# Second mixture of experts: three moves of work in VectorE's, ScalarE's and SyncE's orders

## The chip, the cores and the metric

The kernel runs on one core of a Trainium2 chip. The metric is the device time of one launch in microseconds (us), the median of several runs. The engines are TensorE (PE; its weight loads are shown as PEld), VectorE (DVE), ScalarE (ACT), GpSimd (POOL) and SyncE (SP), which here only issues DMAs. A name with a q behind it (DVEq, PEldq, SPq) is the instruction sequencer of that engine. "L1170" is line 1170 of the kernel.

## The reference

Three stages follow each other. An attention over q, k, v (2 x 8 heads x 768 positions x 64) gives x of 1536 rows x 512. A first mixture adds four experts over all rows, `p[:, e] * (relu(x @ w1[e]) @ w2[e])`, hidden size 1024. The second mixture is sparse:

```
skip_score = x @ w_skip;  do_compute = skip_score > 0;  out = x.copy()
logits = xc @ w_gate;     e_idx = argmax(logits);  gate_w = softmax(logits)[e_idx]
for e in range(8):
    h = relu(xc[mask] @ w1[e]);  y[mask] = gate_w[mask] * (h @ w2[e])
out[do_compute] = xc + y
```

So about half of the rows go to one of 8 experts each, and which row goes where is known only at run time. Everything is float32.

## The kernel before, in words

The change touches the second mixture alone. During the last group of the first mixture the kernel chooses an expert per row and scatters one entry per chosen row (its number and gate weight) into a list in DRAM (`send_entries`, L575, POOL, 12 indirect DMAs). The list has columns of 64 entries, and each is one tile; a tile is of one expert. This input gives 14 tiles: experts 0 to 3 have one tile each, expert 4 five (tiles 4 to 8), experts 5 and 6 one each, expert 7 three (tiles 11 to 13). Each tile holds its 64 rows as 128 half rows.

A tile's work goes through the engines as follows:

- POOL gathers the rows of tile i by an indirect DMA from `x1_rows` (L579) into one of six buffers `xg`, and later scatters the finished rows to `out` (L583). Behind the scatter of tile i stands the gather of tile i+5.
- DVE copies gathered rows into `x_in` (`rows_in`, L1175), PE transposes them (`next_rows`, L1488), and DVE copies the transposed rows to `xt2` (`copy_x`, L1136).
- PE multiplies by the expert's first weights (`layer1`, L1506), ACT applies the relu (`relu_h`, L788), PE transposes the result (`turn_h`, L1513), ACT copies it (`copy_ht`, L792), PE multiplies by the second weights (`layer2`, L1529).
- DVE adds the result, times the gate, to the rows (`add_x`, L1170).

PE works a tile ahead. Its turn i is: `layer1` of tile i, `next_rows` of tile i+1, `layer2` of tile i-1, `turn_h` of tile i. `layer1` of tile i waits for `copy_x(i)` and for its expert's first weights in slot 0.

Weights of an expert are 8 pieces of 512 KB, 4 for each layer. SP loads them (L437) into slot 0 (expert 0) or one of three further slots, and counts each layer that has arrived in `set_ready` (`arrived`, L441). Before use they are copied into slot 0 (`place`): DVE copies 2 of 4 pieces of layer 1 and 3 of 4 of layer 2 (L1188), ACT the others (L799). DVE's turn i before the change is: `add_x(i)`; `place` of layer 2 if tile i+1 has another expert than tile i; the row numbers of tile i+6 (`make_ids`, L1163 to L1165, read from the list); two register loads from a table (L1178, L1181); and, if there are further tiles, `copy_x(i+2)`, `place` of layer 1 if tile i+2 has another expert than tile i+1, and `rows_in(i+3)`. All engines take their instructions in the order written, and a wait holds up all behind it.

At the start of this stage SP issues: all of set 0, layer 1 of set 1, one piece of its layer 2; then (once the last rows of the first mixture are there, `keep(G-1)`, L422) the write of these rows to `x1_rows`, from which POOL gathers tile 0; the three other pieces of set 1; after `gathered[0]` the write of the same rows to `out` (`send_out(G-1)`, L427), two pieces of set 2; after `gathered[1]` everything else. The list, once all entries have landed, is loaded from DRAM by ACT (L784), ahead of ACT's relu of tile 0. `make_ids(1)` on DVE and by it the gather of tile 1 wait for the list.

Of the kernel before, what the change touches and what calls it, by code (L numbers as in the profile page):

```python
# [18 lines left out]
def sparse_attention_moe_moe(nc, q, k, v, dprobs, w1, w2, w_skip, w_gate, v1, v2, out):  # L19
# [27 lines left out]
    NT = N // P  # L47
    G = 4
# [4 lines left out]
    SIDES = 2  # L53
    QT = P // SIDES
    LISTS = N // QT
    TILES = (N + E2 * (QT - 1)) // QT
    SLOTS = 6
# [7 lines left out]
    PIECES = 4  # L65
# [28 lines left out]
    route_list = nc.dram_tensor("route_list", (QT * COLS, 2), F32).ap()  # L94
# [5 lines left out]
    with ExitStack() as ctx:  # L100
# [3 lines left out]
        def sem(name):  # L104
            return ctx.enter_context(nc.semaphore(name))
# [104 lines left out]
        lst = a1[:, o:o + 2 * COLS].rearrange("p (c e) -> p c e", e=2)  # L210
# [34 lines left out]
        def keys_of(a):  # L245
# [23 lines left out]
        x1_out, x1_kept = sem("x1_out"), sem("x1_kept")  # L269
        x1_last = sem("x1_last")  # L270
        x1_tr, x1t_ok, logit_ok = sem("x1_tr"), sem("x1t_ok"), sem("logit_ok")
        r_dve, shifted, r_exp, hot_ok, sum_ok, rank_ps, count_ps = (
            sem("r_dve"), sem("shifted"), sem("r_exp"), sem("hot_ok"), sem("sum_ok"), sem("rank_ps"), sem("count_ps"))
        entry_ok, entries_out, list_in, table_ok = (
            sem("entry_ok"), sem("entries_out"), sem("list_in"), sem("table_ok"))
# [7 lines left out]
        r1_done, relu_ok, ht_done, ht_ok, r2_done, y_ok = (  # L283
            sem("r1_done"), sem("relu_ok"), sem("ht_done"), sem("ht_ok"), sem("r2_done"), sem("y_ok"))
# [10 lines left out]
        def _(sp):  # L295
# [42 lines left out]
            def w1_piece(src, c):  # L338
                return src[c * P:(c + 1) * P, :]

            def w2_piece(src, c):
                return src[2 * c * P:2 * (c + 1) * P, :].rearrange("(j p) d -> p j d", p=P)

            def two(dst):
                return dst.rearrange("p (j d) -> p j d", j=2)
# [72 lines left out]
            def keep(g):  # L418

                sp.wait_ge(acc_ok, 2 + GR * (G * (E1 - 1) + g + 1))  # L420
                rows, src = rows_of_group(g)
                sp.dma_start(x1_rows[rows].rearrange("(t p) d -> p t d", p=P), src).then_inc(x1_kept, 16)  # L422

            def send_out(g):

                rows, src = rows_of_group(g)
                sp.dma_start(out[rows].rearrange("(t p) d -> p t d", p=P), src).then_inc(x1_out if g < G - 1 else x1_last, 16)  # L427

            def slot_of(e):
                return 1 + (e - 1) % AHEAD if e else 0  # L430

            def load_set(e, layer, pieces=range(PIECES)):

                for c in pieces:
                    dst = wset[:, slot_of(e), (PIECES * layer + c) * PIECE:(PIECES * layer + c + 1) * PIECE]
                    src = w2_piece(v2[e], c) if layer else w1_piece(v1[e], c)
                    sp.dma_start(two(dst) if layer else dst, src).then_inc(set_in[slot_of(e)][layer], 16)  # L437

            def arrived(e, layer):
                sp.wait_ge(set_in[slot_of(e)][layer], 16 * PIECES * (1 + (e - 1) // AHEAD))  # L440
                sp.sem_inc(set_ready, 1)  # L441
# [18 lines left out]
            load_set(0, 1)  # L460
            load_set(1, 0)

            load_set(1, 1, range(1))
            keep(G - 1)
            load_set(1, 1, range(1, PIECES))
            arrived(1, 0)
            sp.wait_ge(gathered[0], 16)
            send_out(G - 1)
            load_set(2, 0, range(2))
            arrived(1, 1)  # L470

            sp.wait_ge(gathered[1], 16)
            load_set(2, 0, range(2, PIECES))
# [9 lines left out]
            tiles = sp.value_load(table[0:1, 0:1], min_val=1, max_val=TILES)  # L483
# [139 lines left out]
        def _(act):  # L623
# [133 lines left out]
            def route_exp(g):  # L757
                act.wait_ge(shifted, g + 1)
                nc.scalar.activation(t8[1][:, g * GR:(g + 1) * GR, :], t8[0][:, g * GR:(g + 1) * GR, :], ACT.Exp).then_inc(r_exp, 1)


            for g in range(G):
                c = G * (E1 - 1) + g
# [11 lines left out]
            for t in range(GR * (G - 1), NT):  # L775
                route_copy(t)
            route_exp(G - 1)

            act.wait_ge(x1_kept, 16 * (G - 1))
            act.wait_ge(x1_out, 16 * (G - 1))  # L780
            act.wait_ge(x1_tr, NT)
            act.wait_ge(entries_out, 16 * NT)
            for j in range(SIDES):
                act.dma_start(lst[j * QT:(j + 1) * QT, :, :].rearrange("p c e -> p (c e)"), route_list.rearrange("(p c) e -> p (c e)", p=QT)).then_inc(list_in, 16)  # L784

            def relu_h(i):
                act.wait_ge(r1_done, i + 1)
                nc.scalar.activation(h2, ps[:, 0, 0:FQ], ACT.Relu).then_inc(relu_ok, 1)  # L788
# [23 lines left out]
            tiles = act.value_load(table[0:1, 0:1], min_val=1, max_val=TILES)  # L812
# [20 lines left out]
        def _(dve):  # L833
# [265 lines left out]
            e = E1 - 1  # L1099
# [5 lines left out]
            for g in range(G):  # L1105
                c = G * e + g
# [27 lines left out]
            def copy_x(i):  # L1134
                dve.wait_ge(x_tr, i + 1)
                nc.vector.tensor_copy(xt2, ps[:, 4, 0:DQ]).then_inc(x_ok, 1)  # L1136
# [25 lines left out]
            def make_ids(i, k):  # L1162
                col = dve.value_load(table[0:1, bass.ds(i + COL_OF, 1)], min_val=0, max_val=COLS - 1)  # L1163
                nc.vector.tensor_scalar(id_of[:, k:k + 1], lst[:, bass.ds(col, 1), 0], side[:, 0:1], None, ALU.add).then_inc(id_ok, 1)
                nc.vector.tensor_copy(gate_of[:, k:k + 1], lst[:, bass.ds(col, 1), 1]).then_inc(gate_ok, 1)  # L1165

            def add_x(i, k):
                dve.wait_ge(r2_done, i + 1)
                dve.wait_ge(gate_ok, i)
                nc.vector.scalar_tensor_tensor(out=xg[k % SLOTS], in0=ps[:, 2, 0:DQ], scalar=gate_of[:, k:k + 1], in1=xg[k % SLOTS],  # L1170
                                               op0=ALU.mult, op1=ALU.add).then_inc(y_ok, 1)

            def rows_in(k, uses):
                dve.wait_ge(gathered[k % SLOTS], 16 * uses)
                nc.vector.tensor_copy(x_in, xg[k % SLOTS]).then_inc(rows_ok, 1)  # L1175

            def set_at(i):
                return dve.value_load(table[0:1, bass.ds(i + SET_OF, 1)], min_val=0, max_val=E2 - 1)  # L1178

            def waits_at(i):  # L1180
                return dve.value_load(table[0:1, bass.ds(i + WAIT_OF, 1)], min_val=0, max_val=AHEAD)  # L1181

            def place(then, at, layer):

                dve.wait_ge(set_ready, 2 * then + 1 + layer)
                for c in range(W2_DVE if layer else W1_DVE):
                    cols = slice((PIECES * layer + c) * PIECE, (PIECES * layer + c + 1) * PIECE)
                    nc.vector.tensor_copy(wset[:, 0, cols], wset[:, bass.ds(at, 1), cols].rearrange("p o c -> p (o c)")).then_inc(  # L1188
                        w2_by_dve if layer else w1_by_dve, 1)

            dve.wait_ge(table_ok, 1)
            tiles = dve.value_load(table[0:1, 0:1], min_val=1, max_val=TILES)
# [22 lines left out]
            fourth, at_fourth = set_at(3), waits_at(3)  # L1215
            def turn(i, ago, now, then, at_now, at_then):

                add_x(i, i)
                with dve.If(ago < now):
                    place(now, at_now, 1)  # L1220
                make_ids(i + SLOTS, i + SLOTS)
                beyond, at_beyond = set_at(i + 3), waits_at(i + 3)
                if i + 1 < TILES:
                    with dve.If(tiles > i + 1):

                        copy_x(i + 2)
                        with dve.If(now < then):
                            dve.wait_ge(r1_done, i + 2)
                            place(then, at_then, 0)
                        rows_in(i + 3, 1 + (i + 3) // SLOTS)  # L1230
                        turn(i + 1, now, then, beyond, at_then, at_beyond)
            turn(1, second, third, fourth, at_third, at_fourth)


# [360 lines left out]
```

## Time and profile before

| | before |
|---|---|
| median of 3 runs | 815.03 us (813.95 to 815.23) |
| profiled execution | 812.8 us, span 811.1 us |
| PE busy | 743.6 us, 92% of the span |
| DVE busy | 286.5 us, 35% |
| ACT busy | 204.6 us, 25% |
| POOL busy | 68.5 us, 8% |
| mean granted TensorE clock | 0.972 |

The second mixture takes the span from about 630 us on. "Busy" is the time in which an instruction of the engine was running; the granted clock is 1.00 at TensorE's full 2.4 GHz and 0.50 at 1.2 GHz, and a value between is a mean over a stretch.

### The profile page before, as it was taken

To read this page: it belongs to the slowest core of one execution; us is meant where nothing else is said; L and a number is where in the kernel's file an instruction comes from. 1 tells how busy PE (TensorE), PEld (TensorE's weight loads), DVE (VectorE), ACT (ScalarE), POOL (GpSimd) and SP (SyncE) were. 2 spreads that over 40 slices of the span, in tenths; PEclk is the share of its full clock that TensorE was granted. 3 is DMA by queue.
4 is the path that set the end of the run, shared out by engine and by line. 5 is a ranking of instruction groups with operands and counts; after the bars stand their busy time and mean duration, and the time that the engine had idled before them with its cause. 6 is when DMAs were issued, how large, how long until landed. Compare 5 with 4: busy or idle time off the path is not lost.

```text
span 811.1 us, 12549 instructions
## 1 busy us (share of the span) xinstructions
PE 743.6 (92%) x4608; PEld 608.9 (75%) x4609; DVE 286.5 (35%) x818; ACT 204.6 (25%) x498; POOL 68.5 (8%) x97
## 2 busy tenths in 40 slices
PE   5699999999999999999999999999998778778675
PEld 4588888989989899898898998989897333333233
DVE  4987664524222122341121432232322542211421
ACT  3654454523211011230110311202020132112210
POOL 2530000000000000000000000010101331211210
PEclk9899999999999999999999999999999698999898
DMA  9893612103220000330000020202029599920000
GB/s 206 197 218 88 131 43 57 44 34 108 99 72 1 1 0 0 104 104 0 0 0 0 31 72 1 78 1 78 33 80 344 179 363 396 399 100 19 8 2 19
DMA packets 76947, 75.22 MB, mean 93 GB/s; under 512 B 54088, under 2 KB 54364, under 8 KB 76512
## 3 DMA queue, kind: packets, MB, share of 16 engines
q1 hardware_dynamic: 74080, 69.72, 27.9%
q0 software_dynamic: 2656, 4.66, 1.9%
q8 instruction: 27, 0.44, 0.2%
q10 hardware_dynamic: 160, 0.20, 0.1%
q14 instruction: 24, 0.20, 0.1%
HBM read 66.82 MB, written 8.24 MB: 93 GB/s over the span
## 4 chain that ended last, share of the span: by engine, by line
PE 87%; DVE 5%; issue 2%; DVEq 2%; ACT 1%; DMA 1%; POOL 0%; ACTq 0%; SPq 0%; POOLq 0%
PE ps L1241 22%; PE ps L1243 22%; PE ps L1242 22%; PE ps L1506 7%; PE ps L1529 7%; PE ps L1303 1%; PE ps L1275 1%; PE ps L1426 1%; PE ps L1289 1%; DVE sets L1188 1%; PE ps L1254 1%; PE ps L1416 1%; DVE acc L887 1%; DVEq L1181 1%; DVEq L1163 1%
## 5 line engine op out<-in xcount | busy, mean ns | idle before, releaser
L1241 PE MATMUL ps<-xt_hi,w_hi 128*128 128x384 f32 (+1 forms) x508 | 173.0, 341 | 0.0
L1243 PE MATMUL ps<-xt_hi,w_lo 128*128 128x384 f32 (+1 forms) x508 | 170.2, 335 | 0.0
L1242 PE MATMUL ps<-xt_lo,w_hi 128*128 128x384 f32 (+1 forms) x508 | 170.1, 335 | 0.0
L707 ACT ACTIVATE h_hi<-ps 128x384 fp32r<-128x384 f32 x128 | 63.0, 492 | 359.1 <-PE ps L1243 358.9
L1241 PE MATMUL ps<-w_hi,h_hi 128*128 128x512 f32 x384 | 151.7, 395 | 0.0
L1243 PE MATMUL ps<-w_hi,h_lo 128*128 128x512 f32 x384 | 150.0, 391 | 0.0
L1242 PE MATMUL ps<-w_lo,h_hi 128*128 128x512 f32 x384 | 149.8, 390 | 0.0
L933 DVE SCALAR_TENSOR_TENSOR h_lo<-ps,h_hi 128x384 fp32r<-128x384 f32 x128 | 71.1, 556 | 167.1 <-ACT h_hi L707 166.9
L1241 PEld LDWEIGHTS ps<-xt_hi,w_hi 128*128 128x128 f32 x508 | 95.4, 188 | 1.7 <-issue 0.8
L1242 PEld LDWEIGHTS ps<-xt_lo,w_hi 128*128 128x128 f32 x508 | 95.5, 188 | 0.5
L1243 PEld LDWEIGHTS ps<-xt_hi,w_lo 128*128 128x128 f32 x508 | 95.4, 188 | 0.0
L1506 PE MATMUL ps<-sets,acc 128*64 128x512 f32 x224 | 61.3, 699 | 34.4 <-DVE sets L1188 17.8
L1243 PEld LDWEIGHTS ps<-w_hi,h_lo 128*128 128x128 f32 x384 | 72.1, 188 | 15.2
L1241 PEld LDWEIGHTS ps<-w_hi,h_hi 128*128 128x128 f32 x384 | 72.1, 188 | 15.0 <-issue 0.8
L1242 PEld LDWEIGHTS ps<-w_lo,h_hi 128*128 128x128 f32 x384 | 72.2, 188 | 14.1
L944 DVE SCALAR_TENSOR_TENSOR acc<-ps,dp,acc 128x512 f32<-128x512 f32 x36 | 27.0, 750 | 140.4 <-PE ps L1243 140.3
L1506 PEld LDWEIGHTS ps<-sets,acc 128*64 128x64 f32 x224 | 17.5, 157 | 69.4 <-issue 48.0
L1529 PE MATMUL ps<-sets,acc 128*64 128x256 f32 x448 | 53.3, 392 | 1.5 <-issue 0.7
L575 POOL DMA_INDIRECT route_list<-entry,slot x12 | 12.1, 1004 | 451.5 <-DVE entry L1096 449.1
L1529 PEld LDWEIGHTS ps<-sets,acc 128*64 128x64 f32 x448 | 32.6, 141 | 18.5 <-issue 4.6
L1170 DVE SCALAR_TENSOR_TENSOR acc<-ps,gate_of,acc 128x256 f32<-128x256 f32 x13 | 6.3, 483 | 97.4 <-PE ps L1529 97.4
L788 ACT ACTIVATE h_rows<-ps 128x512 f32<-128x512 f32 x14 | 8.4, 597 | 90.3 <-PE ps L1506 75.6
(172 smaller groups left out, 623.3 us busy)
## 6 DMA issues: line engine op xcount, KB each, us to landing
sets<-in_moe_w SPq DMA_DIRECT2D x64, 512.0 KB, 7.7
stage<-in_moe_w SPq DMA_DIRECT2D x24, 512.0 KB, 4.0
stage<-in_k SPq DMA_DIRECT2D x16, 192.0 KB, 4.8
acc<-in_v SPq DMA_DIRECT2D x4, 768.0 KB, 6.5
x_rows<-acc SPq DMA_DIRECT2D x4, 768.0 KB, 4.2
out_rows<-acc SPq DMA_DIRECT2D x4, 768.0 KB, 5.1
acc<-in_moe_w POOLq DMA_DIRECT2D x4, 512.0 KB, 4.3
acc<-in_moe_w SPq DMA_DIRECT2D x4, 512.0 KB, 5.7
```

The costliest lines, as they stand in the source:

```text
L575: nc.gpsimd.indirect_dma_start(route_list, bass.IndirectOffsetOnAxis(slot[:, t:t + 1], 0), entry[:, t, :], None, bounds_check=QT * COLS - ...
L707: nc.scalar.activation(h_hi[:, f, :], ps[:, f % 2, 0:GT], ACT.Relu).then_inc(h_hi_ok, 1)
L788: nc.scalar.activation(h2, ps[:, 0, 0:FQ], ACT.Relu).then_inc(relu_ok, 1)
L887: TT(rows[0:VR, 0:left], rows[0:VR, 0:left], rows[0:VR, left:2 * left], ALU.add).then_inc(vsum_step, 1)
L933: nc.vector.scalar_tensor_tensor(out=h_lo[:, f, :], in0=ps[:, f % 2, 0:GT], scalar=0.0, in1=h_hi[:, f, :].bitcast(F32), op0=ALU.max, op1=A ...
L944: nc.vector.scalar_tensor_tensor(out=acc[:, t, :], in0=bank, scalar=dp[:, t, bass.ds(e, 1)], in1=acc[:, t, :], op0=ALU.mult, op1=ALU.add). ...
L1163: col = dve.value_load(table[0:1, bass.ds(i + COL_OF, 1)], min_val=0, max_val=COLS - 1)
L1241: mm(dst, a_hi, b_hi, start=start, stop=False)
L1242: mm(dst, a_hi, b_lo, start=False, stop=False)
L1243: return mm(dst, a_lo, b_hi, start=False, stop=stop)
L1506: last = mm(ps[j * QT:(j + 1) * QT, 0, 0:FQ], xt2[:, from_c:from_c + QT], wset[:, 0, at:at + FQ], start=(c == 0), stop=(c == KC - 1))
L1529: last = mm(ps[j * QT:(j + 1) * QT, 2, 0:DQ], ht2[:, at:at + QT], wset[:, 0, to:to + DQ], start=(f == 0), stop=(f == FC - 1))
```

## The change

Three edits. On SP, two pieces of set 1's layer 2 instead of one are issued ahead of `keep(G-1)`; two pieces of set 2 are issued behind `arrived(1, 0)`, ahead of the wait for the first gather; and SP loads the list, behind `send_out(G-1)`. ACT loads it no more. On DVE, the block with `copy_x(i+2)`, `place` of layer 1 and `rows_in(i+3)` stands ahead of `add_x(i)`, in an If of its own.

```
--- before
+++ after
             load_set(1, 0)
 
-            load_set(1, 1, range(1))
+            load_set(1, 1, range(2))
             keep(G - 1)
-            load_set(1, 1, range(1, PIECES))
+            load_set(1, 1, range(2, PIECES))
             arrived(1, 0)
+            load_set(2, 0, range(2))
+            arrived(1, 1)
             sp.wait_ge(gathered[0], 16)
             send_out(G - 1)
-            load_set(2, 0, range(2))
-            arrived(1, 1)
+
+            sp.wait_ge(x1_kept, 16 * (G - 1))
+            sp.wait_ge(x1_out, 16 * (G - 1))
+            sp.wait_ge(x1_tr, NT)
+            sp.wait_ge(entries_out, 16 * NT)
+            for j in range(SIDES):
+                sp.dma_start(lst[j * QT:(j + 1) * QT, :, :]..., route_list...).then_inc(list_in, 16)
 
             sp.wait_ge(gathered[1], 16)
             load_set(2, 0, range(2, PIECES))
...
             route_exp(G - 1)
-
-            act.wait_ge(x1_kept, 16 * (G - 1))
-            act.wait_ge(x1_out, 16 * (G - 1))
-            act.wait_ge(x1_tr, NT)
-            act.wait_ge(entries_out, 16 * NT)
-            for j in range(SIDES):
-                act.dma_start(lst[j * QT:(j + 1) * QT, :, :]..., route_list...).then_inc(list_in, 16)
-
             def relu_h(i):
...
             def turn(i, ago, now, then, at_now, at_then):
 
+                with dve.If(tiles > i + 1):
+                    copy_x(i + 2)
+                    with dve.If(now < then):
+                        dve.wait_ge(r1_done, i + 2)
+                        place(then, at_then, 0)
+                    rows_in(i + 3, 1 + (i + 3) // SLOTS)
+
                 add_x(i, i)
                 with dve.If(ago < now):
                     place(now, at_now, 1)
...
                 if i + 1 < TILES:
                     with dve.If(tiles > i + 1):
-
-                        copy_x(i + 2)
-                        with dve.If(now < then):
-                            dve.wait_ge(r1_done, i + 2)
-                            place(then, at_then, 0)
-                        rows_in(i + 3, 1 + (i + 3) // SLOTS)
                         turn(i + 1, now, then, beyond, at_then, at_beyond)
```

## Rows read from the trace of the kernel before

**Rows 1.** The page: the chain that ended last, by engine.
```profile
PE 87%; DVE 5%; issue 2%; DVEq 2%; ACT 1%; DMA 1%; POOL 0%; ACTq 0%; SPq 0%; POOLq 0%
```

**Rows 2.** Timeline of PE: start us, us, line, operation, count [idle before, released by].
```profile
657.59 3.65 PE L1506 MATMUL ps<-sets,acc 128*64 128x512 f32 x16 [0.82 <-DVE sets L1188]
669.22 5.35 PE L1506 MATMUL ps<-sets,acc 128*64 128x512 f32 x16 [3.42 <-DVE sets L1188]
695.27 3.65 PE L1506 MATMUL ps<-sets,acc 128*64 128x512 f32 x16 [2.84 <-DVE acc L1136]
702.83 0.66 PE L1513 MATMUL ps<-ident,h_rows 128*128 128x128 f32 x4
706.32 5.35 PE L1506 MATMUL ps<-sets,acc 128*64 128x512 f32 x16 [2.84 <-DVE acc L1136]
718.72 3.65 PE L1506 MATMUL ps<-sets,acc 128*64 128x512 f32 x16 [2.50 <-DVE acc L1136]
740.64 5.35 PE L1506 MATMUL ps<-sets,acc 128*64 128x512 f32 x16 [3.00 <-DVE sets L1188]
754.31 5.35 PE L1506 MATMUL ps<-sets,acc 128*64 128x512 f32 x16 [3.76 <-DVE sets L1188]
791.06 3.65 PE L1506 MATMUL ps<-sets,acc 128*64 128x512 f32 x16 [2.47 <-DVE acc L1136]
```

**Rows 3.** Chain of waits, 701 to 707 us: start us, us, what.
```profile
702.94 0.08 DVE acc L1170
703.02 0.49 issue
...
703.51 0.30 DVEq L1163
...
705.76 0.43 DVE acc L1136
```

**Rows 4.** Chain of waits, pieces of one turn of PE.
```profile
695.27 3.65 PE ps L1506 x16
698.92 0.37 PE ps L1488 x2
699.29 3.63 PE ps L1529 x32
```

**Rows 5.** Stretches: us, busy PE PEld DVE ACT POOL (count), clock, DMA share, GB/s.
```profile
706.30:711.70 5.40, 5.38 (x17) 1.61 (x18) 0.09 (x1) 0.00 (x0) 0.36 (x1) 0.68 1.04 394
718.70:722.40 3.70, 3.68 (x17) 1.19 (x18) 0.09 (x1) 0.00 (x0) 0.72 (x1) 1.00 0.12 37
660.00:715.00 55.00, 42.52 (x252) 19.22 (x250) 13.10 (x33) 11.99 (x16) 9.98 (x9) 0.91 1.02 389
```

**Rows 6.** Timeline of all engines, 660 to 684 us (the weights of tiles 3 and 4).
```profile
666.91 2.00 ACT L799 ACTIVATE sets<-sets 128x1024 f32 x2 [5.03 <-SPq L441]
...
677.96 2.00 ACT L799 ACTIVATE sets<-sets 128x1024 f32 x2 [2.75 <-SPq L441]
678.47 0.66 PE L1513 MATMUL ps<-ident,h_rows 128*128 128x128 f32 x4
678.99 1.88 DVE L1188 COPY sets<-sets 128x1024 f32 x3
681.78 1.30 DVE L1188 COPY sets<-sets 128x1024 f32 x2
683.00 0.27 DVE L1175 COPY acc<-acc 128x256 f32<-128x256 f32 x1
```

**Rows 7.** PE's sequencer, line 1534, 701 to 707 us: register loads, first and last start.
```profile
L1534 PEldq TENSOR_LOAD <-table x2: 296/298/299, 701.3 to 706.5; - x2
```

**Rows 8.** Timeline of the start of the stage, all engines.
```profile
631.76 1.06 POOL L579 DMA_INDIRECT acc<-x_rows,first_ids  x1 [10.94 <-issue]
635.69 3.65 PE L1506 MATMUL ps<-sets,acc 128*64 128x512 f32 x16
641.40 1.15 ACTq L784 DMA_DIRECT2D acc<-route_list  x2
642.39 1.29 DVE L1188 COPY sets<-sets 128x1024 f32 x2 [3.12 <-issue]
642.67 0.60 ACT L788 ACTIVATE h_rows<-ps 128x512 f32<-128x512 f32 x1 [14.72 <-issue]
645.24 0.21 DVE L1164 TENSOR_SCALAR id_of<-acc,side 128x1 uint32 x1 [1.56 <-DMA acc<-route_list]
```

**Rows 9.** Landing of line 579's gathers (us); the first gather's; the SyncE queue's wait.
```profile
DMA to landing us min/median/max: 2.1/2.9/6.5
...
acc<-x_rows,first_ids POOLq DMA_INDIRECT x1, 2.3
...
SPq L437 <- DMA acc<-x_rows,id_of: 12.8, 1, 12.8
```

**Rows 10.** Stretches around the first gather, columns as in rows 5.
```profile
624.60:628.00 3.40, 1.76 (x13) 1.39 (x12) 0.83 (x7) 0.82 (x2) 0.00 (x0) 1.00 0.78 230
632.00:634.00 2.00, 2.00 (x7) 0.91 (x6) 1.57 (x11) 0.00 (x0) 1.24 (x2) 0.50 0.29 105
```

More of the change, by code:

```diff
@@ L461, in _ @@
             load_set(1, 0)
-            load_set(1, 1, range(1))
+            load_set(1, 1, range(2))
             keep(G - 1)
-            load_set(1, 1, range(1, PIECES))
+            load_set(1, 1, range(2, PIECES))
             arrived(1, 0)
+            load_set(2, 0, range(2))
+            arrived(1, 1)
             sp.wait_ge(gathered[0], 16)
             send_out(G - 1)
-            load_set(2, 0, range(2))
-            arrived(1, 1)
+            sp.wait_ge(x1_kept, 16 * (G - 1))
[3 more added lines that the diff above has]
+            for j in range(SIDES):
+                sp.dma_start(lst[j * QT:(j + 1) * QT, :, :].rearrange("p c e -> p (c e)"), route_list.rearrange("(p c) e -> p (c e)", p=QT)).then_inc(list_in, 16)
             sp.wait_ge(gathered[1], 16)
@@ L777, in _ @@
             route_exp(G - 1)
-            act.wait_ge(x1_kept, 16 * (G - 1))
-            act.wait_ge(x1_out, 16 * (G - 1))
-            act.wait_ge(x1_tr, NT)
-            act.wait_ge(entries_out, 16 * NT)
-            for j in range(SIDES):
-                act.dma_start(lst[j * QT:(j + 1) * QT, :, :].rearrange("p c e -> p (c e)"), route_list.rearrange("(p c) e -> p (c e)", p=QT)).then_inc(list_in, 16)
             def relu_h(i):
```

## The prediction

> **What bounds the kernel now.** I read the page's chain first: 87% of the span is PE, and the only other engine with some per cent is DVE with its sequencer [rows 1]. The change lies in the second mixture, so I read PE's timeline there. The reader should see idle time ahead of `layer1` and nowhere else in a turn: 2.5 to 3.8 us in the eleven turns of tiles 3 to 13, always released by DVE, either its `copy_x` (L1136) or its weight copies (L1188) [rows 2]. Inside a turn `layer1`, `next_rows`, `layer2` and `turn_h` follow without a gap [rows 4].
>
> The chain of one such gap shows why [rows 3]. `layer2` of tile 4 ends at 702.92. Then DVE does `add_x` (0.08 us of it, then 0.49 us of branch), the register load of L1163 at 703.51, the row numbers, two more register loads, and only at 705.76 `copy_x`, which takes 0.43 us; 0.12 us later PE starts. The transposed rows that `copy_x` takes were ready before `layer2` began, at 699.29 [rows 4]. So it is an order problem on one engine: the copy was possible 3.6 us before the add's input existed and stands 2.8 us behind it.
>
> The gap costs twice. `layer1` takes 3.65 us at granted clock 1.00 (2.4 GHz) and 5.35 us where the stretch reads 0.68, a mix of 2.4 and 1.2 GHz [rows 2, 5]. In these turns all `layer1` behind 3.0 us of idle or more are slow, those behind 2.50 or less are fast, and at 2.84 both occur [rows 2]. The slow one costs 1.70 us.
>
> A second bound holds the first part of the stage: from 660 to 715 us the DMA engines move 389 GB/s at full share, which are the weights [rows 5]. ACT's copy for tile 4 starts at 677.96, released by SP's report that the set has arrived [rows 6]. After that tile no expert is new until tile 9, when all weights are there.
>
> **Part 1, VectorE's order.** The steady turn first. Without a gap a turn of PE is 3.65 + 0.37 + 3.63 + 0.57 us (the last: `turn_h` ends at 703.49, `layer2` at 702.92) = 8.22 us [rows 2, 4]. Does anything take the gap's place? `copy_x(i+2)` now runs as soon as its transposes are there, with `layer2` (3.63) and `turn_h` (0.57) of cover. Where an expert changes, two weight copies (1.30) and `rows_in` (0.27) follow [rows 6]; with the copy that is about 2.0 us plus some branches, less than 3.63, so `add_x` isn't late. Were it late, its readers are `layer2` of the next tile and the scatter: `layer2` comes 0.57 + 3.65 + 0.37 = 4.6 us later, which covers `add_x` (0.48) and the three copies of layer 2 (1.88) [rows 6]. I cost this at nothing. ACT's copies start right behind its relu and take 2.0 us, under `layer2` [rows 6].
>
> What is late next is PE itself. Its sequencer must read a register before `layer1`; in the trace that load runs at 701.3, 1.6 us before `layer2` has ended, so the sequencer is well ahead of the array [rows 7]. I take 0 for it. The nearest row for the upper end is the shortest gap of any later `layer1`, 0.82 us at tile 2 (there it has another releaser) [rows 2]: 0 to 0.82 us a turn.
>
> From `layer1` of tile 5 (695.27) to that of tile 13 (791.06) lie 8 turns and 95.79 us [rows 2]. At 8.22 they are 65.8. Saved: 30.0 us. Behind 791.06 nothing changes: 811.1 - 791.06 = 20.0 us stay.
>
> **The turns that the weights bound.** Tile 4 can't start before its set has arrived at 677.96. Before, DVE's two copies came only at 681.78, behind `add_x`, and `layer1` at 682.5. Now DVE stands waiting for the set: its first copy takes 0.65 to 0.69 us (1.30 for two), so `layer1(4)` starts at about 678.75, and the second DVE piece and ACT's two keep ahead of it. PE is ready earlier: tile 3 starts in the same way 0.75 us behind its own set (ACT began that one at 666.9), at 667.7, and ends its turn 8.2 us later at 675.9. That leaves a gap of 2.8 us ahead of tile 4, just where fast and slow both occur. I take half of 1.70, 0.85. So `layer1(5)` starts at 678.75 + 8.22 + 0.85 = 687.8 instead of 695.27: 7.5 us saved. What tiles 1 to 3 gain is lost again in that wait. Does the stream of weights keep its pace? SP reloads a slot only when its set has been placed, and each placing is earlier or as early as before, so yes.
>
> The rule of the Trainium skill that bears here (TensorE: Matmul & The Clock Gate, section "Why this matters for your kernels") is that idle gaps between bursts of matmuls drop the array to half rate. The trace agrees, with 0.68 behind the long gaps and 1.00 behind the short [rows 2, 5]; by the rule no `layer1` from tile 5 on is slow, which is also what the 8.22 says.
>
> The Trainium skill also speaks against the new order a little: Advanced Engine Details and Errata, section "Control Flow Timing", gives about 108 ns for a compare-and-branch, and DVE now has one If more in a turn. The sum would be the same by it, since DVE has over 2 us to spare in a turn, but it would be 1.3 us more were DVE's order still on the path.
>
> **Part 2, ScalarE and the list.** ACT waited 14.7 us for the entries and the list's issue, and its relu of tile 0 came at 642.67, 3.3 us after `layer1` had ended at 639.3 [rows 8]. Without it `layer2(0)` ends some 4 us earlier, but then PE waits for tile 1's rows. These come by a chain through DVE: list landed, `make_ids(1)` at 645.24 after 1.56 us of waiting for the list [rows 8], gather, and `gathered[1]`, which SP also awaits (12.8 us) before the rest of the weights [rows 9]. So the list's landing sets the start of the whole stream, and a shift s there moves everything behind it by s. SP issues as ACT did, behind the same entries; but the two pieces that were in flight with the last entries are gone by then, so the entries land sooner. At most 1.56 us are to be had: then `make_ids` follows the weight copies at 642.39 + 1.29. At least 0 of it, if the entries' own latency rules.
>
> **Part 3, two pieces ahead of the first gather, one more ahead of the rows' write.** 1.05 MB more go through the engines before the gather of tile 0 (issued at 631.76). The reader should see two things: from 624.6 to 628 they moved 230 GB/s instead of 389, so 0.54 MB of this fit in the hole; and from 632 to 634, where the gather ran, they were nearly idle at 105 [rows 5, 10]. The remaining 0.5 MB is 1.3 us of traffic beside the gather. That gather landed after 2.3 us, the range over all is 2.1 to 6.5 [rows 9]. Cost: 0 to 4.4 us; I take 0.8, near the low end, since the traffic ends as the gather begins. It delays `copy_x(0)`, the table and DVE's first weight copies, hence `make_ids(1)`. Together s = 1.5 - 0.8 = 0.7 us earlier, with ends 1.6 and -2.9 (1.5 - 4.4).
>
> The Trainium skill (DMA: Bandwidth & Descriptors, section "Issuing engines are not separate DMA queues") says that DMAs of all issuing engines end on the same 16 engines and interleave. By it the list's move to SP gives nothing in itself, and the early pieces can only hurt the gather; no row here shows the list from SP.
>
> **Sum.** 811.1 - 30.0 - 7.5 - 0.7 = 772.9 us of span. The profiled execution was 1.7 us longer than its span and the median of the runs 2.2 us above it, so I expect 772.9 + 3.9 = 776.8 us.
>
> **Rivals.**
> A, PE's own control shows: up to 0.82 us a turn, over nine turns 7.4 us, 784. For it: no trace shows back-to-back turns. Against: the register load at 701.3 [rows 7].
> B, the start is lost: the first gather meets the pieces and takes up to 6.5 us [rows 9]. s = -2.9 instead of 0.7: 780.4. For it: the gather had an idle window, which is filled now [rows 10].
> C, another engine holds each turn, such as ACT's copies or a late `add_x`, and only half of the steady saving stays: 776.8 + 15 = 792. Against: the sums above leave each engine over 1 us.
> D, slower than before: `rows_in(i+3)` now stands ahead of `add_x(i)`, and gathers are issued only behind scatters, which wait for `add_x`. That closes a loop over two turns: `add_x` 0.5, scatter and gather issue about 2.3, landing, `rows_in` 0.3. At the longest landing, 6.5 [rows 9], it is 9.6 us against 16.4 us for two turns, so it is hidden. It decides from a landing of 13.3 us, and makes the kernel slower only when two turns pass the old 23.9 (95.79 / 8 x 2): at a landing of 25 us, 14.05 a turn, 8 x 2.1 = 17 us more, 832. Nothing in the trace lands so late.
> E, the move does nothing, because `copy_x` still waits for something that comes with the end of `layer2`. Its input stands ahead of `layer2` in PE's order, so 815 would need that reading to be wrong.
>
> **How the numbers follow.** Forecast 68% (772 to 781 by itself), A 12%, B 9%, C 8%, D 1%, E 2% (half of it slower by the added start cost). The range 772 to 788 takes the forecast, A, B and the unknown terms' bounds: all good ends give 811.1 - 30.0 - 8.4 - 1.6 + 3.9 = 775, and a runs' median 2 to 3 us nearer the profile leads to 772; all bad ends give 776.8 + 7.4 + 3.6 + 0.85 = 788.6. A measurement of this kernel can tell about 0.2% from no change. Faster by more: 0.97; within: 0.01; slower: 0.02.
>
> **What would show it.** In the profile after, `layer1` of tiles 5 to 13 starts under 0.3 us behind `turn_h`, 8.2 us apart, all 3.65 us long. DVE's L1136 is released by PE's L1488, before L1170 in each turn. Ahead of tile 4 a gap of 2 to 3 us ends with DVE's weight copy, released by SP's arrival. The relu of tile 0 starts by 640.5. `make_ids(1)` comes at 643.5 to 645. Wrong would be: gaps over 1 us from tile 5 on; a first gather landing over 1 us later; or a DMA stream that ends later than before.

## The result and the profile after

The changed kernel takes 775.27 us (774.4 to 775.4, 4 runs) against 815.04 us before: a ratio of 0.9512, 95% interval 0.9496 to 0.9529. The forecast was 776.8. The profiled execution took 775.32 us, with a span of 773.6.

TensorE's timeline after, in the columns of [rows 2]:

```profile
657.50 3.65 PE L1506 MATMUL ps<-sets,acc 128*64 128x512 f32 x16 [0.66 <-DVE sets L1187]
...
669.31 5.35 PE L1506 MATMUL ps<-sets,acc 128*64 128x512 f32 x16 [3.60 <-DVE sets L1187]
...
680.28 3.65 PE L1506 MATMUL ps<-sets,acc 128*64 128x512 f32 x16 [1.05 <-DVE sets L1187]
...
688.42 3.65 PE L1506 MATMUL ps<-sets,acc 128*64 128x512 f32 x16
...
753.57 3.65 PE L1506 MATMUL ps<-sets,acc 128*64 128x512 f32 x16
```

These are the `layer1` of tiles 2, 3, 4, 5 and 13. From tile 5 on there is no bracket: no idle time, and each of the nine takes 3.65 us. From 688.42 to 753.57 there are 65.15 us for 8 turns, 8.14 each, where [rows 2] had 95.79. One turn in the timelines of PE and DVE shows the new order:

```profile
700.52 3.67 PE L1529 MATMUL ps<-sets,acc 128*64 128x256 f32 x32
700.63 0.42 DVE L1135 COPY acc<-ps 128x256 f32<-128x256 f32 x1 [3.27 <-PE ps L1488]
...
704.24 0.48 DVE L1169 SCALAR_TENSOR_TENSOR acc<-ps,gate_of,acc 128x256 f32<-128x256 f32 x1 [2.99 <-PE ps L1529]
704.71 3.65 PE L1506 MATMUL ps<-sets,acc 128*64 128x512 f32 x16
```

The copy of the next rows (L1135, L1136 before) runs at the start of `layer2` and not behind the sum (L1169, L1170 before) as in [rows 3]; DVE has idle time ahead of both.

What sets tile 4 is in the chain of waits (start us, us, what), and in two stretches with the columns of [rows 5]:

```profile
669.86 9.50 DMA sets<-in_moe_w
...
679.38 0.02 SPq L441
...
679.53 0.71 DVE sets L1187
...
680.28 3.65 PE ps L1506 x16
```

```profile
669.30:674.60 5.30, 5.29 (x17) 1.46 (x17) 3.14 (x8) 2.69 (x4) 2.23 (x2) 0.68 1.05 398
688.00:760.00 72.00, 72.00 (x478) 34.35 (x479) 22.91 (x63) 20.21 (x28) 18.15 (x17) 1.00 0.45 168
```

The weights land, SP reports, DVE places the first piece, TensorE starts 0.75 us behind. Tile 3's `layer1` is at 0.68 of the clock behind 3.60 us of idle; from 688 to 760 us TensorE is busy throughout at 1.00.

The start of the stage after, in the timeline of all engines and in the DMA view (engine, count, KB each, median us to landing) from 633 to 648 us:

```profile
635.22 1.06 POOL L586 DMA_INDIRECT acc<-x_rows,first_ids  x1 [11.41 <-issue]
...
642.12 1.17 SPq L477 DMA_DIRECT2D acc<-route_list  x2
642.89 0.60 ACT L787 ACTIVATE h_rows<-ps 128x512 f32<-128x512 f32 x1 [11.49 <-PE ps L1506]
...
647.19 0.21 DVE L1163 TENSOR_SCALAR id_of<-acc,side 128x1 uint32 x1
```

```profile
route_list<-entry,slot POOLq DMA_INDIRECT x3, 2.4
acc<-x_rows,first_ids POOLq DMA_INDIRECT x1, 2.9
```

Absolute times mislead here, because the part ahead of this stage, whose code is the same, ended 3.0 us later in this execution: the write of the last rows (L422) was issued at 627.65, before at 624.66. The difference is there already at the first of these four writes (513.27 against 510.29), ahead of every edited instruction. All marks below are therefore counted from that issue ("mark 0"). In these terms the gather of tile 0 is issued at 7.6 instead of 7.1 and lands after 2.9 us instead of 2.3 [rows 9]; the last entries land 2.4 us after their issue, and before 5.1 (the same view, 630 to 648 us of the kernel before); the relu of tile 0 starts at 15.2 instead of 18.0; `make_ids(1)` at 19.5 instead of 20.6 [rows 8]; ACT's placing for tile 4 at 51.9 instead of 53.3 [rows 6].

Tile 1's `layer1` also starts 2.9 us earlier (24.2 instead of 27.1). The `layer2` of tile 0 ahead of it, in PE's timeline, before and after:

```profile
645.23 5.57 PE L1529 MATMUL ps<-sets,acc 128*64 128x256 f32 x32 [0.73 <-issue]
```

```profile
644.99 3.67 PE L1529 MATMUL ps<-sets,acc 128*64 128x256 f32 x32 [0.73 <-issue]
```

Before, the late relu left TensorE idle for 4.06 us, this `layer2` then ran slowly (granted clock 0.61 from 643.4 to 650.8 us) and ended at 26.1, and it held back tile 1. After, the clock stays at 1.00, `layer2` ends at 21.0, and tile 1 waits for its gather instead.

From mark 0 to the end are 145.95 us against 186.44: 40.5 us gained, of which the late start took 3.0 back in this pair of executions. They split so: 9.84 by the start of `layer1(5)`, 30.64 in the eight turns, 0.01 behind.

### The profile page after: what moved, and what is told of

Same layout as the page of the kernel before. It is cut to its first block, busy times and chain, and to the rows that moved or that the text cites. A ratio compares the mean times of both kernels' runs of the same rounds, so it can differ in the third digit from the quotient of the medians.

```text
span 773.6 us, 12562 instructions
## 1 busy us (share of the span) xinstructions
PE 734.4 (95%) x4608; PEld 608.4 (79%) x4609; DVE 286.9 (37%) x818; ACT 204.8 (26%) x498; POOL 69.2 (9%) x97
## 4 chain that ended last, share of the span: by engine, by line
PE 88%; DMA 6%; DVE 3%; issue 1%; DVEq 0%; ACT 0%; SPq 0%; POOL 0%; POOLq 0%
PE ps L1241 23%; PE ps L1243 23%; PE ps L1242 23%; PE ps L1529 5%; PE ps L1506 5%; DMA sets<-in_moe_w 3%; PE ps L1303 2%; PE ps L1275 1%; PE ps L1426 1%; PE ps L1289 1%; DMA acc<-in_moe_w 1%; DMA acc<-stage 1%; PE ps L1254 1%; PE ps L1513 1%; PE ps L1416 1%
## 5 line engine op out<-in xcount | busy, mean ns | idle before, releaser
L1243 PEld LDWEIGHTS ps<-w_hi,h_lo 128*128 128x128 f32 x384 | 72.1, 188 | 15.2
L1506 PE MATMUL ps<-sets,acc 128*64 128x512 f32 x224 | 52.9, 615 | 6.1 <-DVE sets L1187 5.3
L1529 PE MATMUL ps<-sets,acc 128*64 128x256 f32 x448 | 51.4, 382 | 1.5 <-issue 0.7
L1529 PEld LDWEIGHTS ps<-sets,acc 128*64 128x64 f32 x448 | 31.9, 137 | 17.2 <-issue 3.0
L1506 PEld LDWEIGHTS ps<-sets,acc 128*64 128x64 f32 x224 | 15.5, 140 | 33.9 <-issue 26.2
L1187 DVE COPY sets<-sets 128x1024 f32 x35 | 22.2, 685 | 13.7 <-SPq L441 10.6
L798 ACT ACTIVATE sets<-sets 128x1024 f32 x21 | 21.3, 1049 | 13.0 <-SPq L441 11.0
```

Of the source, the lines that this page charges most:

```text
L798: nc.scalar.activation(wset[:, 0, cols], wset[:, bass.ds(at, 1), cols].rearrange("p o c -> p (o c)"), ACT.Copy).then_inc(w2_by_act if laye ...
L1243: return mm(dst, a_lo, b_hi, start=False, stop=stop)
L1506: last = mm(ps[j * QT:(j + 1) * QT, 0, 0:FQ], xt2[:, from_c:from_c + QT], wset[:, 0, at:at + FQ], start=(c == 0), stop=(c == KC - 1))
L1529: last = mm(ps[j * QT:(j + 1) * QT, 2, 0:DQ], ht2[:, at:at + QT], wset[:, 0, to:to + DQ], start=(f == 0), stop=(f == FC - 1))
```

## The experiments

Marks in us from mark 0, from the timeline of each run's profiled execution. "set 4 placed" is the start of the first copy of tile 4's first weights, "5 to 13" goes from the start of `layer1(5)` to that of `layer1(13)`, "to the end" from mark 0 to the end of the span:

```
                       make_ids(1)  set 4 placed  layer1(4)  layer1(5)  5 to 13  to the end  median us
before                    20.6         53.3          57.9       70.6      95.79    186.4      815.0
changed                   19.5         51.9          52.6       60.8      65.15    146.0      775.27
changed, once more        19.5         52.6          53.4       61.5      65.15    146.7      775.11
e1 VectorE alone          20.4         52.7          53.4       62.9      65.14    148.0      775.07
e2 queues alone           19.6         52.4          56.2       67.3      97.35    184.7      813.21
e3 late pieces            20.5         53.9          54.6       62.8      65.15    147.9      777.16
e4 list by ScalarE        19.4         53.1          53.9       62.0      65.14    147.2      774.15
e5 two more pieces        19.6         50.7          51.4       61.3      65.15    146.5      773.24
e6 four more pieces       19.6         47.2          48.7       56.9      65.15    142.0      770.21
e9 copy alone             19.8         52.5          59.3       67.5      78.74    166.2      792.6
e10 e6, kept busy         19.6         48.9          49.7       57.8      65.15    143.0      771.79
e11 five row buffers      19.4         51.6          52.4       60.5      67.18    147.5      774.67
```

**Which part did it.** e1 takes the kernel before and changes only VectorE's turn:

```
+                with dve.If(tiles > i + 1):
+                    copy_x(i + 2)
+                    ...place(then, at_then, 0); rows_in(...)
                 add_x(i, i)
```

> Only VectorE's new order; SyncE's and ScalarE's orders as before. Theory (the order on VectorE gives nearly all; the queue edits only let the weights arrive 1.5 us earlier): weights arrive as in the kernel before, so layer1 of tile 4 comes 1.5 us later than in the changed kernel, and the gap ahead of it is near 2.8 us, which may cost 1.7 us of half clock: 776.8 to 778.5 us. Rival 1 (the queue edits give nothing): 775.3. Rival 2 (they give the 3 us by which tile 1 came earlier): 778.3 or more, with every layer1 from tile 1 on later by 3 us.

It measured 775.07 us, ratio 0.9511 (0.9498 to 0.9525). That is the changed kernel's, so VectorE's order gives all that can be seen. The traces show `make_ids(1)` 0.9 us later than in the changed kernel; but the set of tile 4 is placed at 52.7, and the two profiles of the changed kernel itself have 51.9 and 52.6. The stream's own spread is as large as the gain, so rival 1 stands, in the sense that the gain isn't measurable in the run times. From mark 0 to the end the one profile of e1 is 1.4 to 2.1 us longer than the two of the changed kernel, 1.3 us of it in a `layer1(4)` of 4.99 us behind a gap of 2.91. But its mark 0 lies 2.4 us earlier (625.28 against 627.65 and 627.63), which hides this in the whole time.

e2 is the opposite: the changed kernel with VectorE's old turn.

> Only SyncE's and ScalarE's edits; VectorE's turn as before. Theory: where VectorE's order still sets the turns and not the weights, the whole 3 us by which tile 1 comes earlier survive to the end: 812.0 us. Rival (these edits are worth the same in either order): 1.5 us, 813.5. Rival (nothing): 815.0. All gaps of 2.5 us and more ahead of layer1 stay.

813.21 us, ratio 0.998 (0.9966 to 0.9994): 0.5 to 2.8 us faster than before. `layer1(1)` came 2.9 us earlier, as expected, but only 1.8 us of it are left at the end of the profile: which of the remaining gaps drop the clock varies from execution to execution. The interval ends just short of the theory's 3.0 and holds its rival's 1.5; the size stays open.

**The queue edits one by one**, each with the new VectorE order. e3 moves the pieces back, e4 the list:

```
e3:  load_set(1, 1, range(1)); keep(G - 1); load_set(1, 1, range(1, PIECES)); arrived(1, 0)
     gathered[0]; send_out(G - 1); load_set(2, 0, range(2)); arrived(1, 1); ...list by SyncE
e4:  SyncE as changed, without the list; ScalarE loads it where it did
```

> The changed kernel, but the weight pieces stand where they stood before (one piece ahead of the rows' write, set 2's two pieces behind send_out); the list still comes from SyncE. Theory (the list came early because the two pieces no longer ran beside the last entries): the last entries land 5 us after their issue instead of 2.4, the weights' stream starts 1 to 2 us later, 776.5 to 778. The first gather lands about 0.6 us sooner. Rival (the issuer was the point, not the pieces): 775.3.

> The changed kernel, but ScalarE loads the list, as before; the pieces stay early. Theory: the list lands at the same time, ScalarE's relu of tile 0 comes about 0.5 us later, and tile 1's rows are later than that anyway: 775.3, no difference. Rival (freeing ScalarE was worth the 3 us of tile 1): up to 778.

e3: 777.16 us, 0.9538 (0.9518 to 0.9559). e4: 774.15 us, 0.9493 (0.9479 to 0.9506). The mechanism of e3 is as expected: the entries land after 5.1 us again, the first gather after 2.3, and the list is issued at 16.8 instead of 14.5. In e4 nothing is lost. e3 and e1 differ only in the issuer of the list and have the same `make_ids(1)`, yet e3 is 2.1 us slower. In their profiles this lies ahead of the stage: mark 0 is at 627.50 in e3 and at 625.28 in e1, and from there to the end they take 147.9 and 148.0 us, though set 4 comes later in e3 (53.9 against 52.7).

The changed kernel, e1, e3 and e4 are all four combinations of early or late pieces and of the list by SyncE or ScalarE. Early pieces are 1.9 us faster with SyncE's list (changed against e3) and 0.9 us with ScalarE's (e4 against e1); ScalarE's list is 1.1 us faster with early pieces (e4) and 2.1 us with late ones (e1). Each pair's intervals overlap, so neither effect is clear of noise.

**The weights set tile 4.** e5 and e6 issue two or four more pieces behind the list, ahead of the wait for the second gather, into the hole that DMA has there:

```
             for j in range(SIDES): ...the list...
+            load_set(2, 0, range(2, PIECES))
+            load_set(2, 1, range(2))          # e6 alone
             sp.wait_ge(gathered[1], 16)
```

> The changed kernel, but the other two pieces of set 2's first layer are issued right behind the list instead of behind the second gather. Theory (the arrival of set 4's first layer starts tile 4, and all behind follows in unbroken turns): 1.05 MB ahead of the wait is 2.7 us at 389 GB/s, so all from tile 4 on comes 2.7 us earlier: 772.6 us, or up to 1.4 more if the gap ahead of tile 4 (about 2.8 us) lowers the clock. Rival (the second gather loses by the traffic what the stream gains): 775 to 777.

> As before it, but four pieces: set 2's first layer and half of its second. Theory: 5.4 us earlier, 769.9 us, since TensorE itself would be ready for tile 4 only 1 us before the set. The traffic (2.1 MB, 5.4 us from the list's issue) now ends about as the second gather lands, which may cost 1 to 2 us of it: up to 772. Rival (that gather is delayed as much as the stream gains): 775 or more.

e5: 773.24 us, 0.9483 (0.9463 to 0.9503). e6: 770.21 us, 0.9449 (0.9431 to 0.9466). The changed kernel beside them: 775.11 us, 0.9502 (0.9481 to 0.9523). e6 gives about the 5 us that the stream's rate says (4.9; 5.4 were expected), and it is the fastest version here. Its timeline of TensorE, `layer1` of tiles 2, 3 and 4:

```profile
658.50 3.65 PE L1507 MATMUL ps<-sets,acc 128*64 128x512 f32 x16 [0.81 <-DVE sets L1188]
...
666.64 3.65 PE L1507 MATMUL ps<-sets,acc 128*64 128x512 f32 x16
...
674.78 3.65 PE L1507 MATMUL ps<-sets,acc 128*64 128x512 f32 x16
```

No gap is left from tile 2 on. e5 in its profile lost most of its gain at tile 4: a gap of 3.47 us and a `layer1` of 5.35. Its 773.24 us fits the expectation, but its interval overlaps the changed kernel's.

e10 is e6 with `idle_turns(12)` ahead of tile 1's transposes:

> The version with four more pieces ahead of the second gather, and twelve short matmuls of unused data on TensorE between layer2 of tile 0 and the transposes of tile 1, where it idles about 3.4 us. Theory (TensorE is the bound from tile 1 on, and layer1 of tile 1 ran partly at half clock after the idle time, 4.83 instead of 3.65 us): 1.2 us less, 769.0 us. Rival (the clock there costs nothing): 770.2.

771.79 us, 0.947 (0.9457 to 0.9482): no gain. `layer1(1)` took 3.66 us instead of 4.83 and tile 3 began 1.1 us earlier, both as expected, but then TensorE waited for the weights again at tile 4:

```profile
677.27 3.65 PE L1507 MATMUL ps<-sets,acc 128*64 128x512 f32 x16 [2.02 <-DVE sets L1188]
```

In e6 the first piece for tile 4 was in place only some 0.8 us before TensorE needed it, so the two are nearly even there, and what TensorE gains waits for the stream. In e10 the set also came 1.7 us later than in e6 (48.9 against 47.2) with the same order of loads, so part of this wait is the stream's; why it was slower I don't know.

**What must stand ahead of the sum.** e9 moves the copy alone; the weights and `rows_in` stay behind:

```
                 with dve.If(tiles > i + 1):
                     copy_x(i + 2)
-                    with dve.If(now < then): ...place(then, at_then, 0)
-                    rows_in(i + 3, 1 + (i + 3) // SLOTS)
                 add_x(i, i)
```

> The changed kernel, but only the copy of the next rows stands ahead of the sum; the placing of the first layer's weights and rows_in stand behind the row numbers as before. Theory: turns without a new expert (tiles 5 to 8, 12, 13) stay 8.14 us apart; ahead of tiles 9, 10 and 11 a gap of about 3.3 us comes back, with 1.7 us of half clock in most, and tile 4 starts about 3.5 us later: 789 to 793 us. Rival (the copy was all that mattered): 775.3.

792.6 us, 0.9704 (0.9681 to 0.9727), as expected. Its timeline at tiles 9 and 10, where the expert changes again:

```profile
728.16 1.47 DVE L1187 COPY sets<-sets 128x1024 f32 x2 [1.50 <-issue]
728.91 3.65 PE L1506 MATMUL ps<-sets,acc 128*64 128x512 f32 x16 [2.96 <-DVE sets L1187]
...
740.47 5.35 PE L1506 MATMUL ps<-sets,acc 128*64 128x512 f32 x16 [3.35 <-DVE sets L1187]
```

The gap comes back exactly in the turns that place weights: 2.96, 3.35 and 3.36 us ahead of tiles 9, 10 and 11, where the kernel before had 3.00, 3.76 and 3.38. In these turns the copy alone is worth next to nothing.

**How much cover each place has.** The same six extra copies of 128x1024 stand ahead of the copy (e7) or ahead of the sum (e8):

```
e7:   dve.wait_ge(x_tr, i + 3); filler(6); copy_x(i + 2)
e8:   rows_in(...); filler(6)
      add_x(i, i)
```

> The changed kernel with six extra VectorE copies of 128x1024 (one behind the other, 0.69 us each and some link time, about 4.6 us in all, of data that nothing uses) in every turn, behind the wait for the transposes and ahead of the copy of the next rows. Theory (the copy has 4.2 us of cover under layer2 and turn_h): a gap of about 1.1 us in each turn from tile 5 on, 1.8 where weights are placed: 785 to 788 us. Rival (VectorE's work now costs its full length a turn): 40 us more, 815.

> The same six copies, but behind rows_in and ahead of the sum. Theory (a late sum is covered by the next layer1): the sum comes some 2 to 3 us later in each turn and TensorE doesn't wait: 775.3 to 777 us. Rival (a late sum holds layer2 or the gathers): 783 or more.

e7: 784.47 us, 0.963 (0.9615 to 0.9645). e8: 783.02 us, 0.9612 (0.9597 to 0.9628). e7 is near what was expected (785 to 788); the six took 4.33 us:

```profile
700.55 4.33 DVE L1217 COPY stage<-stage 128x1024 f32<-128x1024 f32 x6 [3.02 <-PE ps L1494]
...
704.92 0.42 DVE L1135 COPY acc<-ps 128x256 f32<-128x256 f32 x1
...
705.48 3.65 PE L1512 MATMUL ps<-sets,acc 128*64 128x512 f32 x16 [0.78 <-DVE acc L1135]
```

So 4.33 us of work cost 0.84 us in such a turn (8.98 instead of 8.14): the rest was covered. Where weights are placed the gap was 1.29 to 1.42 us. e8 was expected to cost at most 2 us and cost 7.8. From tile 5 to tile 10 the theory held, 8.14 us a turn. TensorE waited elsewhere, ahead of `layer2` of tiles 3, 10 and 13 among others:

```profile
685.70 5.36 PE L1535 MATMUL ps<-sets,acc 128*64 128x256 f32 x32 [2.32 <-DVE sets L1187]
...
746.10 3.67 PE L1535 MATMUL ps<-sets,acc 128*64 128x256 f32 x32 [1.09 <-DVE sets L1187]
...
770.12 3.67 PE L1535 MATMUL ps<-sets,acc 128*64 128x256 f32 x32 [3.08 <-DVE acc L1169]
```

A late sum makes the second layer's weights late, since they are placed behind it. At tile 3 DVE had also stood waiting for tile 4's first set (1.10 us) before it came to the extra copies and the sum. At the end no `layer1` is left to cover the sum. My claim "a late sum costs nothing" is true only as far as the placing behind it fits too.

**The loop over the gathers (rival D).** e11 has five row buffers:

```
-    SLOTS = 6
+    SLOTS = 5
```

> The changed kernel with five row buffers instead of six, so that the gather of tile i+4 stands behind the scatter of tile i and rows_in(i+4) stands ahead of the sum of tile i+1: the loop over gathers, scatters and sums closes over one turn. Theory: sum 0.5, scatter and gather issue 2.4, landing 2.9, rows_in 0.3 make 6.1 us, under the 8.14 of a turn, and a late sum is covered: 775.3 to 776.5 us. Rival (the loop of rival D is near deciding): a turn of 9 us or more while weights load, 780 or more.

774.67 us, 0.9505 (0.9489 to 0.952): the same time. But the loop does decide while the weights load. The DVE and POOL rows of one pass (`rows_in` is L1174):

```profile
697.12 0.48 DVE L1169 SCALAR_TENSOR_TENSOR acc<-ps,gate_of,acc 128x256 f32<-128x256 f32 x1
...
699.80 1.03 POOL L586 DMA_INDIRECT acc<-x_rows,id_of  x1 [0.31 <-issue]
...
705.46 0.29 DVE L1174 COPY acc<-acc 128x256 f32<-128x256 f32 x1 [5.45 <-DMA acc<-x_rows,id_of]
705.67 0.48 DVE L1169 SCALAR_TENSOR_TENSOR acc<-ps,gate_of,acc 128x256 f32<-128x256 f32 x1
```

From sum to sum are 8.55 us, with a landing of 5.6, over the 8.14 of a turn. Three turns took 8.42, 8.59 and 9.46; tiles 5 to 13 are 67.2 us instead of 65.15. My expectation had used the quiet landing of 2.9. The same run time doesn't speak against this: from mark 0 to the end e11 took 147.5 us, 0.8 to 1.6 more than the two profiles of the changed kernel, and its mark 0 lay 2.4 us earlier (625.20). So the loop costs about 2 us in tiles 5 to 13, and in this profile the drift of the part ahead hides it.

## Why the prediction was right, step by step

*The gap ahead of `layer1` is one of order on VectorE, and nothing takes its place.* Right. Predicted 8.22 us a turn and 30.0 saved; measured 8.14 and 30.6. TensorE's own register load hides: rival A's 0.82 us a turn didn't show. Rival C (half the gain, 792) and E (none, 815) fell with the result, and e1 shows that VectorE's order alone is enough.

*Tile 4 is set by its weights.* Right, shown by the chain and by e6. The terms were off in two ways that cancel in part. The set came 1.4 us earlier and not 0.7; e1 and e4 show that this much lies within the stream's spread. And I charged half of 1.70 us for the clock at tile 4. The slow `layer1` came at tile 3, behind 3.60 us of idle where I had worked with 1.9 (I had not moved tiles 1 and 2 by the 3 us that they gained). That ate the gap ahead of tile 4 (1.05 us), and tile 4 ran fast. So by `layer1(5)` 9.84 us were gained, where 7.5 + 0.7 stood.

*ScalarE's free queue gains nothing at the end.* Right with VectorE's new order (e4, e1), but I had tile 1 gain nothing at its start either, and it gained 2.9 us. I had missed that `layer2(0)` ran at a low clock behind the late relu: it ended 5.1 us earlier, not 4, and in the kernel before tile 1's rows had been waiting for it. e4 has the same start of tile 1 (24.1) with the list on ScalarE, and e3 has 25.3 with the list on SyncE but late, so either an early list or a free ScalarE gives most of it. With VectorE's old order the edits give 0.5 to 2.8 us (e2): there no wait for weights swallows them.

*The early pieces: first gather 0.8 us later, entries sooner.* Mechanism right: it landed 0.6 us slower and was issued 0.5 later, 1.1 in all and so just past the 1 us that I had set as a sign of being wrong (other versions with early pieces land it in 3.2 to 3.4 us: e2, e4, e11). The entries landed in 2.4 us instead of 5.1, which outweighs it. Its net worth is not settled: 1.9 us by e3 against the changed kernel, 0.9 by e1 against e4, neither clear of noise.

*The sum.* Predicted span 772.9, measured 773.6: in the stage 40.5 us instead of 38.2, less 3.0 of an earlier part that ended later. The 2.2 us between the profile of before and its median, which I added, weren't there after: that median is as its profile. So the terms hold to 2.3 us, and that the forecast is only 1.5 us off is in part luck: the drift of 3.0 stands against the other two errors.

*The clock.* The Trainium skill (TensorE: Matmul & The Clock Gate, "Why this matters for your kernels") has idle gaps drop the array to half rate. The trace agrees from tile 5 on, 1.00 with no gap. It isn't sharp: in e2 gaps of 3.38 and 3.00 us were followed by a `layer1` of 3.65 us, and one of 2.50 by 5.35. In e3 a gap of 1.77 us was enough, after a stretch at 1.00 (665 to 669 us):

```profile
671.09 5.35 PE L1506 MATMUL ps<-sets,acc 128*64 128x512 f32 x16 [1.77 <-DVE sets L1187]
```

So my reading of [rows 2], fast behind 2.50 us or less and slow behind 3.0 or more, holds only for that trace. In these runs a gap between 1.8 and 3.4 us can be priced only as a chance.

## What to carry to other kernels

Where one engine serves two consumers in a pipeline, put the work whose input is ready first, ahead of a wait for later work, and move with it everything that the same consumer waits for (the copy without the weights gave 22 us of 40). After such a move look for the next bound where transfers feed the pipeline: here TensorE gave back what it had gained at tile 1 in a wait for weights, and 2 MB more in an idle stretch of DMA were worth 5 us. Count marks from an event just ahead of the stage, in every version that is compared, because the part ahead drifts (mark 0 lies between 624.7 and 627.7 us here) by as much as a small edit is worth: in the profiles it hides the cost of five row buffers, and it is all of the difference between e3 and e1.

## What was not expected of the hardware

In e11 an indirect gather of 128 rows of 1 KB landed in 2.2 to 2.9 us once the weights were there (from 717 us on, DMA share 0.11 or less) and in 5.6 to 6.9 while they streamed (issued from 689 to 709 us; 397 GB/s). The stream's own pace varied: from `make_ids(1)` to the placing of set 4 the same code took 32.3 and 33.1 us, and other versions with the same pieces up to 33.7.
